# One product a tile for the group sums, one for turn and slots of kv, and both y halves of two experts at once

## The chip, the cores and the metric

The kernel runs on one core of one Trainium2 chip. The metric is device time in microseconds (us). A core has five engines that run side by side, each taking its own instructions in program order: PE (TensorE, matmuls into PSUM; PEld are its weight loads), DVE (VectorE), ACT (ScalarE), POOL (GpSimd) and SP (SyncE, which here issues nearly all transfers). They wait for each other on semaphores.

## The reference, cut to what matters

```python
kv  = einsum('bhsd,bhse->bhde', k, v)          # 8 batches, 8 heads, 576 rows, 64 wide
out = einsum('bhsd,bhde->bhse', q, kv)
x   = out / sqrt(mean(out*out, -1) + 1e-6) * g_norm     # -> 4608 tokens x 512
logits = x @ phi                                # 32 slots, 4 for each of 8 experts
d = softmax over tokens of logits;  slot_input = d.T @ x
h = relu(slot_input[e] @ w1[e]);  slot_out[e] = h @ w2[e]     # 512 -> 1024 -> 512
c = softmax over slots of logits;  return c @ slot_out
```

All operands are fp32. A matmul with fp32 operands shows in the trace as two instructions, which the text calls passes.

## The kernel before, in words

**Order.** The kernel writes out one program order by hand. `Order.add` records every operation with what it reads and writes, finds for each the operations on other engines that it must wait for, and `emit` gives them to the engines (so every instruction has line 214). In PSUM the unit of that bookkeeping is a whole bank: an operation that writes into a bank waits for every earlier read of that bank by another engine in the same 32 partitions. An engine never overtakes its own order.

**PSUM.** In the first phase the eight banks are shared out as `o` (two buffers of two banks, the products of a tile), `kv` (banks 4 and 5), `m` (one buffer, bank 6) and `s` (one buffer, bank 7). Tag `m` serves by turns `group_max_T` (the turned group maximum), `group_exp_PE` (the maximum spread to all partitions), the warm-up products of `fill_wide`, and `psT`.

**kv.** For each batch `Kv.products` and `Kv.borders` form k'v in PSUM, ACT copies it to `kvT`, and `Kv.slots` turns it (a transpose for each half g) and multiplies it with the gated phi (`gphi`, one matmul for each half). ACT copies both results into `bd`, the right operand of the next batches' products (for batch 0 DVE copies the second).

**Loop over 36 tiles of 128 tokens.** `products(T)` gives out and logits of a tile in one product with `bd`; ACT squares and copies it (`sq`, `part`, `xall`); DVE sums squares (`ms`), makes the inverse root with three small steps (`newton`) and adds the logits; POOL scales. Tiles form six groups G of six. When a group's logits are there, DVE takes their maximum (`group_max`), PE turns it (`group_max_T`), DVE reduces it (`group_max_row`), and two tiles later `group_exp` makes `d`. Then come `group_sum(G, i)` for i = 0, 2, 4, one in each of three tiles' turns. Each call multiplies d' with x of two tiles: four matmuls of 32 rows, two for the even and odd column blocks of each tile, one in each quarter of the output partitions, 258 columns each (two blocks of 128 and two ones columns, so that the sums of d come out too). After i = 4 DVE adds the result `pS` to `acc`, scaled by `alpha`.

**Tail.** After tile 35, groups 4 and 5 are left. The order there is: on DVE `group_max(G)` of the last group; then the sums of group 4 with their add into `acc`; then `fill_wide` (four matmuls of 512 fp32 columns, into tag `m`, whose result nobody reads); then `group_max_T`, `group_max_row`, `group_diag`, `group_exp` and the sums of group 5; then `psT`, which folds `acc` with `fold`, and the scaling into `sTe`.

**Experts and output.** `expert_h(e)` multiplies `sTe` with w1; `expert_y(e, hf)` multiplies the turned h with half hf of w2's columns (256) into bank hf of `pY`, eight matmuls of 32 rows in four quarters. After all `expert_y(e, 0)`, `gather(0)` copies the sums out, `mix(0)` adds the quarters with `sel`, and `output` forms the left half of the result and stores it; then the same for the right half. Weights stream in all through the kernel as their places become free.

Of the kernel before, what the change touches and what calls it, by code (L numbers as in the profile page):

```python
# [20 lines left out]
GROUPS = (6,) * 6  # L21
# [3 lines left out]
NX = 14  # L25
# [6 lines left out]
LATE = 6  # L32
# [253 lines left out]
def soft_moe_linear_attention(nc, first_in, kv_in, q0_in, q1_in, kv4_in, kv5_in, t3_in, w_in, out):  # L286


    const = Const(nc)
# [2 lines left out]
    arena = const.tile([P, HEAD + ARENA], F32, name="arena")  # L292
    phi_sb = arena[:, :128].rearrange("p (g w n) -> p g w n", g=2, w=2)
    g2 = arena[:, 128:129]
    xall = const.tile([P, NX, 4, 129], F32, name="xall")
    xflat = xall.rearrange("p i j n -> p (i j n)")


# [60 lines left out]

    nc.scalar.preload_act_table_set("natural_log_exp_and_others")  # L360

    ident = const.tile([P, P], F32, name="ident")
    make_identity(nc, ident)
    ones = const.tile([P, P], F32, name="ones")
    nc.gpsimd.memset(ones, 1.0)
    zeros = const.tile([P, 256], BF16, name="zeros")
    nc.vector.memset(zeros, 0.0)
    stepped = const.tile([P, 16], F32, name="stepped")
    small = const.tile([P, 4], F32, name="small")
    eps = small[:, :1]  # L370
    nc.gpsimd.memset(eps, EPS_RMS)
    fold = const.tile([P, 2, 64], F32, name="fold")
    nc.vector.tensor_reduce(out=fold[:, 0], in_=ident.rearrange("p (g n) -> p n g", g=2), axis=AX.X, op=ALU.add)
# [3 lines left out]
    gphi = const.tile([P, 2, 2, 2, NS], F32, name="gphi")  # L377
    nc.gpsimd.memset(gphi, 0.0)
    for i in range(2):
        lo = 64 * i  # L380
# [5 lines left out]
    nc.gpsimd.memset(xall[:, :, :, 128:129], 1.0)  # L386
    nc.gpsimd.tensor_copy(out=fold[:, 1], in_=fold[:, 0])
    xts = [xall[:, (i + 6) % NX] for i in range(NX)]

    L = const.tile([P, NT + len(GROUPS) + 1, NS], F32, name="logits")  # L390
# [2 lines left out]
        return T + T // GROUPS[0] + 1  # L393

    run_max = [small[:, 1 + i : 2 + i] for i in range(2)]
    acc = const.tile([P, 258], F32, name="acc")
# [4 lines left out]
    ps = pool(o=(2, 0, 2), kv=(2, 4), m=(1, 6), s=(1, 7))  # L401


    class Kv:


        def __init__(self, b, tag="kv", bufs=None):
            self.b = b
            self.bd = bds[b % 2]
            t = ps.tile([P, 2, 512], F32, tag=tag, name=f"kvp{b}_{tag}", bufs=bufs)  # L410
            self.pkv = t[:, :, :128].rearrange("p w (g d) -> p w g d", g=2)
            self.pT = t[:, 0, 128:384].rearrange("p (g n) -> p g n", g=2)
            self.pM = t[:, 1, 128:384].rearrange("p (g h w n) -> p g h w n", g=2, h=2, w=2)

        def products(self, r):
            g, w = divmod(r, 2)
# [30 lines left out]
        def slots(self, gs):  # L447
            kvT = [self.kvT[:, k].rearrange("p w d -> p (w d)") for k in range(len(gs))]
            for t, g in zip(kvT, gs):
                nc.tensor.transpose(self.pT[:, g], t, ident)  # L450
            for t, g in zip(kvT, gs):
                nc.tensor.matmul(self.pM[:, g], lhsT=t, rhs=gphi[:, g], start=True, stop=True)
            a, z = gs[0], gs[-1] + 1
            for i in range(2):
                lo = 64 * i
                nc.scalar.copy(
                    self.bd[lo : lo + 64, 2 * a : 2 * z, 32 + lo : 96 + lo],
                    self.pT[lo : lo + 64, a:z].rearrange("p g (h d) -> p (g h) d", h=2),
                )
# [123 lines left out]
    g0 = [sum(GROUPS[:G]) for G in range(len(GROUPS) + 1)]  # L583
# [37 lines left out]
    def group_exp(G):  # L621
# [6 lines left out]
        if G > 0:  # L628
            alphas[G] = wk.tile([P, 1], F32, tag="alpha", name=f"alpha{G}")
            nc.scalar.activation(alphas[G], run_max[G % 2], AF.Exp, scale=-1.0, bias=run_max[(G - 1) % 2])  # L630

    def group_sum(G, i):

        if i == 0:
            sums[G] = ps.tile([P, 258], F32, tag="s", name=f"pS{G}")
        pS = sums[G]
        for a in range(2):
            x = xts[(g0[G] + i + a) % NX]
            for j in range(2):
                at = 64 * a + 32 * j  # L640
                nc.tensor.matmul(
                    pS[at : at + 32].rearrange("p (j n) -> p j n", n=129),
                    lhsT=ds[G][:, i + a],
                    rhs=x[:, j::2],
                    start=i == 0,
                    stop=i == GROUPS[G] - 2,
                )
        if i == GROUPS[G] - 2:
            if G == 0:
                nc.vector.tensor_copy(out=acc, in_=pS)  # L650
            else:
# [32 lines left out]
    def fill(n, cols=256, home=None):  # L684

        if not n:
            return
        t = home if home is not None else ps.tile([P, 2, 512], F32, tag="o", name="fill", bufs=2)[:, 1]
        for i in range(n):
            nc.tensor.matmul(  # L690
                t[:, :cols].rearrange("p (a n) -> p a n", n=256),
                lhsT=zeros[:, :P],
                rhs=zeros.unsqueeze(1).to_broadcast([P, cols // 256, 256]),
                start=True,
                stop=True,
            )
# [26 lines left out]
    for T in range(NT - 2):  # L723
# [32 lines left out]
            group_exp_PE(pb_at[T])  # L756
            d_at[T + 1] = pb_at[T]
        if T in sums_at:
            todo_sums += [(sums_at[T], i) for i in range(0, GROUPS[sums_at[T]], 2)]
        if todo_sums:  # L760
            group_sum(*todo_sums.pop(0))
        if T in loads_behind:
# [12 lines left out]
    logits_adds(s - 2)  # L775
    scale_x(s - 2)
    group_exp(G - 1)
    todo_sums += [(G - 1, i) for i in range(0, GROUPS[G - 1], 2)]
    mean_square(s - 1)
    oZ = products(Z)  # L780
    root(s - 1, tail_ps[:, 0, 256 : 256 + H])
# [21 lines left out]
    group_exp(G)  # L803
    scale_o(Z, oZ, True)
    fill(LATE_FILL[2], home=tail_ps[:, 1], cols=512)
    for i in range(0, GROUPS[G], 2):
        group_sum(G, i)
    fill(LATE_FILL[3], home=tail_ps[:, 1], cols=512)

# [1 line left out]
    sTe = wk.tile([P, NE * 4 * NS], F32, tag="sq", name="sTe")  # L811
    nc.gpsimd.memset(sTe, 0.0)
    psT = ps.tile([P, P + 1], F32, tag="m", name="psT")
    for j in range(2):
        nc.tensor.matmul(
            psT[:, 64 * j : 64 * j + 64], lhsT=acc[:, 129 * j : 129 * j + 128], rhs=fold[:, 0], start=True, stop=True
        )
    nc.tensor.matmul(
        psT[:, 128:129], lhsT=fold.rearrange("p a n -> p (a n)"), rhs=acc[:, 128:129], start=True, stop=True
    )  # L820
    fill(LATE_FILL[4], home=tail_ps[:, 1], cols=512)
    mine = psT[:, :P].rearrange("p (j e k) -> p e j k", j=4, k=SPE)
# [37 lines left out]
    ]  # L860

    hTs = {}
    pY = ps.tile([P, 2, 512], F32, tag="y", name="pY", bufs=1)

    def w2_unit(e, hf):
        first = NE - LATE
        if e < first:
            return e, 8 * hf
        return first + hf * LATE // 2 + (e - first) // 2, 8 * (e % 2)

    def expert_h(e):
        ph = ps.tile([P, 2, 512], F32, tag="m", name=f"ph{e}")[:, 0, :256]
# [16 lines left out]
    def expert_y(e, hf, cs=range(8)):  # L889
        u, at = w2_unit(e, hf)  # L890
        for c in cs:
            j = c % 4
            nc.tensor.matmul(
                pY[32 * j : 32 * j + 32, hf, :256],
                lhsT=hTs[e][:, c],
                rhs=w_block("w2", u, at + c),
                start=e == 0 and c < 4,
                stop=e == NE - 1 and c >= 4,
            )

    zs = {}
# [3 lines left out]
    def halves(name, srcs):  # L907
        t = [wk.tile([P, 2, P], F32, tag="part", name=f"{name}_{f}", bufs=3)[:, f] for f in range(2)]
        nc.vector.tensor_copy(out=t[0], in_=srcs[0])
        nc.scalar.copy(t[1], srcs[1])  # L910
        return t

    def gather(hf):
        ys[hf] = halves(f"y{hf}", [pY[:, hf, f * P : f * P + P] for f in range(2)])

    def mix(hf):
        pz = [ps.tile([P, 2, 512], F32, tag="m", name=f"pz{hf}_{f}")[:, 0, :P] for f in range(2)]
        for f in range(2):
            nc.tensor.matmul(pz[f], lhsT=sel.rearrange("p a n -> p (a n)"), rhs=ys[hf][f], start=True, stop=True)
        zs[hf] = halves(f"z{hf}", pz)  # L920

    def step_over(n):
# [172 lines left out]
```

How the kernel before makes its waits and increments, by code:

```python
    def emit(self):  # L203
        nc = self.nc
        counters = {e: nc.alloc_semaphore(f"done_{e}") for e in ENGINES[:4]}
        sems = list(counters.values())
        counts = dict.fromkeys(counters, 0)
        for op in self.ops:
            method, args, kwargs = op.call
            engine = getattr(nc, op.engine)
            *before, last = sorted(op.waits, key=lambda w: w.i) or [None]
            for w in before:
                engine.wait_ge(w.sem, w.value)
            inst = getattr(engine, method)(*args, **kwargs)
            if last is not None:
                inst.wait_op(last.sem, last.value, "sem-ge")
            if op.dma:
                op.sem, op.value = nc.alloc_semaphore(f"dma_{op.i}"), 16
                sems.append(op.sem)
                inst.then_inc(op.sem, 16)
            elif op.signals:
                counts[op.engine] += 1
                op.sem, op.value = counters[op.engine], counts[op.engine]
                inst.then_inc(op.sem, 1)
        for op in self.ops:
            if op.dma and not op.signals:
                nc.sync.wait_ge(op.sem, 16)
        numbers = sorted(s.num for s in sems)
        assert numbers == list(range(numbers[0], numbers[-1] + 1))
        nc.sync.sem_clear(range(numbers[0], numbers[-1] + 1))
```

## Time and profile before

| | |
|---|---|
| time, median of 3 runs | 172.08 us (171.82 to 172.19) |
| time of the profiled execution | 171.97 us |
| its span, first to last instruction | 170.6 us |
| PE busy | 149.0 us (87%), 1832 instructions |
| DVE, ACT, POOL busy | 86.6, 89.0, 59.6 us |
| moved by DMA | 71.65 MB, 420 GB/s on the mean |

An engine's busy time is the union of its instructions' spans, and the spans of pipelined matmuls overlap, so the distance from one start to the next says what a matmul costs. Idle time of an engine is put down to what ended it.

### The profile page before, as it was taken

How to read it: one execution, taken by the hardware profiler on the slowest of the kernel's cores; microseconds unless marked ns; L12 is line 12 of the kernel's file. 1: busy time of each engine (PE TensorE's matmuls, PEld its weight loads, DVE VectorE, ACT ScalarE, POOL GpSimd, SP SyncE). 2: the span in 40 equal slices, each digit the busy share in tenths (PEclk: the TensorE clock that was granted, in tenths of full speed). 3: DMA queues.
4: the chain of work that ended last, by engine and by line, in shares of the span. 5: the costliest groups of instructions: out<-in, count | busy, mean ns of one | idle time of the engine just before them, and what ended most of it. 6: DMA issues, size and time to landing. Idle time of an engine off the chain costs nothing.

```text
span 170.6 us, 4233 instructions
## 1 busy us (share of the span) xinstructions
PE 149.0 (87%) x1832; PEld 105.0 (62%) x1832; DVE 86.6 (51%) x185; ACT 89.0 (52%) x230; POOL 59.6 (35%) x73
## 2 busy tenths in 40 slices
PE   7989696989999899999899998989999989989300
PEld 3468576979778888897697674346655543455000
DVE  1122156284677266762946698823888137218400
ACT  3027576796975886859759864202223045217400
POOL 7000707648357745377382679500000004000000
PEclk9999999999999999999999999999999999999955
DMA  5999999999999999999999999999999999999996
GB/s 186 417 429 421 444 415 439 473 416 452 462 415 421 432 441 430 419 399 451 415 449 407 455 392 421 447 434 415 430 426 442 436 442 392 431 419 434 416 455 277
DMA packets 4365, 71.65 MB, mean 420 GB/s; under 512 B 790, under 2 KB 790, under 8 KB 922
## 3 DMA queue, kind: packets, MB, share of 16 engines
q1 hardware_dynamic: 3994, 71.18, 97.8%
q8 instruction: 14, 0.23, 0.5%
q0 software_dynamic: 352, 0.20, 0.4%
q14 instruction: 5, 0.04, 0.1%
HBM read 61.94 MB, written 9.44 MB: 418 GB/s over the span
## 4 chain that ended last, share of the span: by engine, by line
PE 58%; DMA 13%; ACT 12%; DVE 7%; SPq 2%; issue 1%
PE psum L214 58%; DMA arena<-in_kv_dram 13%; ACT bd L214 3%; ACT sq L214 3%; ACT xall L214 2%; SPq L214 2%; DVE arena L214 1%; DVE logits L214 1%; ACT arena L214 1%; DVE ms L214 1%; ACT part L214 1%; ACT d L214 1%; DVE part L214 1%; ACT r L214 1%; DVE acc L214 1%
## 5 line engine op out<-in xcount | busy, mean ns | idle before, releaser
L214 PE MATMUL psum<-bd,arena 128*128 128x192 f32 (+1 forms) x320 | 56.1, 335 | 1.9 <-ACT bd L214 1.5
L214 PEld LDWEIGHTS psum<-bd,arena 128*128 128x128 f32 (+1 forms) x320 | 45.4, 179 | 8.7 <-ACT bd L214 2.8
L214 DVE TENSOR_REDUCE ms<-sq 128x16 f32<-128x1024 f32 (+1 forms) x19 | 22.1, 1162 | 32.8 <-ACT sq L214 32.5
L214 POOL TENSOR_TENSOR part<-part,r 128x512 f32<-128x512 f32 x17 | 17.8, 1048 | 49.6 <-DVE r L214 49.6
L214 POOL TENSOR_TENSOR xall<-xall,r 128x512 f32<-128x512 f32 x34 | 34.7, 1042 | 0.0
L214 ACT ACTIVATE sq<-psum 128x512 f32<-128x512 f32 x36 | 21.5, 598 | 11.7 <-PE psum L214 11.2
L214 PE MATMUL psum<-arena 128*64 128x64 f32 (+1 forms) x640 | 21.7, 226 | 2.8 <-DMA arena<-in_kv_dram 2.7
L214 PEld LDWEIGHTS psum<-arena 128*64 128x64 f32 (+1 forms) x640 | 19.0, 137 | 8.2 <-DMA arena<-in_kv_dram 3.6
L214 ACT COPY xall<-psum 128x512 f32<-128x512 f32 x34 | 20.6, 606 | 0.0
L214 ACT COPY part<-psum 128x256 f32<-128x256 f32 (+1 forms) x38 | 13.6, 359 | 11.2 <-DVE part L214 10.0
L214 DVE TENSOR_REDUCE logits<-part 128x64 f32<-128x512 f32 (+1 forms) x18 | 17.8, 988 | 0.0
L214 PE MATMUL psum<-logits,part 32*128 32x384 f32 x96 | 13.5, 523 | 1.5 <-ACT arena L214 0.7
L214 PE MATMUL psum<-arena,xall 128*32 128x256 f32 x256 | 14.7, 380 | 0.0
L214 ACT COPY arena<-psum 128x768 f32<-128x768 f32 (+1 forms) x14 | 10.2, 754 | 5.3 <-PE psum L214 5.2
L214 POOL DMA_DIRECT2D out_dram<-arena x2 | 1.2, 589 | 33.4 <-ACT arena L214 33.4
L214 PE MATMUL psum<-arena,sq 128*32 128x256 f32 x224 | 12.7, 379 | 0.2 <-DVE sq L214 0.2
L214 DVE COPY arena<-psum 128x768 f32<-128x768 f32 (+1 forms) x12 | 10.3, 888 | 4.7 <-PE psum L214 4.7
L214 PEld LDWEIGHTS psum<-arena,xall 128*32 128x32 f32 x256 | 8.3, 110 | 6.0 <-issue 1.0
L214 PE MATMUL psum<-xall,d 128*32 128x258 f32 x144 | 10.8, 390 | 0.8 <-ACT d L214 0.8
L214 PEld LDWEIGHTS psum<-logits,part 32*128 32x128 f32 x96 | 6.3, 183 | 7.8 <-ACT arena L214 4.3
L214 ACT COPY bd<-psum 64x128 f32<-64x128 f32 (+1 forms) x32 | 9.9, 309 | 1.6 <-PE psum L214 1.4
L214 PEld LDWEIGHTS psum<-arena,sq 128*32 128x32 f32 x224 | 7.2, 110 | 5.1 <-DVE sq L214 0.5
(80 smaller groups left out, 124.1 us busy)
## 6 DMA issues: line engine op xcount, KB each, us to landing
arena<-in_w_dram SPq DMA_DIRECT2D x4, 4096.0 KB, 23.5
arena<-in_w_dram SPq DMA_DIRECT2D x4, 2048.0 KB, 20.0
arena<-in_t_dram SPq DMA_DIRECT2D x1, 6912.0 KB, 36.1
arena<-in_w_dram SPq DMA_DIRECT2D x2, 3072.0 KB, 22.6
arena<-in_kv_dram SPq DMA_DIRECT2D x2, 2304.0 KB, 23.6
arena<-in_kv_dram SPq DMA_DIRECT2D x1, 4608.0 KB, 42.8
arena<-in_kv_dram SPq DMA_DIRECT2D x1, 3584.0 KB, 32.4
arena<-in_kv_dram SPq DMA_DIRECT2D x3, 1152.0 KB, 12.0
```

What stands on the lines that cost most here:

```text
L214: inst = getattr(engine, method)(*args, **kwargs)
```

## The change

- `xall` loses its ones columns (129 to 128 wide) and with them a memset; `fold` with its reduction and copy goes, and what used it uses `sel`.
- `group_sum` takes one matmul a tile: 32 rows, 512 columns, tile t of the group in quarter t % 4. It is called for i = 0 (four tiles) and i = 4 (two tiles). With i = 4 come three matmuls of two tiles' d (64 rows) with one column of ones into `p1`, a column of tag `m`. Then DVE adds `pS` (now 512 wide) to `acc` and `p1` to a column of `small`.
- `slots` makes turn and slots of a half in one matmul with `turns` (identity beside `gphi`), 256 columns, each half into a bank of its own.
- `psT` takes four matmuls of 32 columns with `sel` in place of two of 64 with `fold`; the one-column matmul stays.
- For experts 0 and 1 `expert_y` takes both halves in one matmul of 512 columns into bank 0; `gather_whole` copies that bank to SBUF on ACT; the other six experts go to bank 1 (hf 0) and bank 0 again (hf 1), and `mix` adds both parts with two matmuls where it had one.

```diff
-    xall = const.tile([P, NX, 4, 129], F32, name="xall")
+    xall = const.tile([P, NX, 4, P], F32, name="xall")
...
+    turns = const.tile([P, 3, P], F32, name="turns")
+    ident = turns[:, 0]
...
-                nc.tensor.transpose(self.pT[:, g], t, ident)
-            for t, g in zip(kvT, gs):
-                nc.tensor.matmul(self.pM[:, g], lhsT=t, rhs=gphi[:, g], start=True, stop=True)
+                nc.tensor.matmul(self.turned[:, g], lhsT=t, rhs=turns[:, : g + 2 : g + 1], start=True, stop=True)
...
+    def add_up(G, part, new):
+        if G == 0:
+            nc.vector.tensor_copy(out=part, in_=new)
+        else:
+            nc.vector.scalar_tensor_tensor(
+                out=part, in0=part, scalar=alphas[G], in1=new, op0=ALU.mult, op1=ALU.add
+            )
...
     def group_sum(G, i):
+        n = GROUPS[G]
         if i == 0:
-            sums[G] = ps.tile([P, 258], F32, tag="s", name=f"pS{G}")
+            sums[G] = ps.tile([P, 512], F32, tag="s", name=f"pS{G}")
         pS = sums[G]
-        for a in range(2):
-            x = xts[(g0[G] + i + a) % NX]
-            for j in range(2):
-                at = 64 * a + 32 * j
+        for t in range(i, min(i + 4, n)):
+            at = 32 * (t % 4)
+            nc.tensor.matmul(
+                pS[at : at + 32],
+                lhsT=ds[G][:, t],
+                rhs=xts[(g0[G] + t) % NX].rearrange("p j n -> p (j n)"),
+                start=i == 0,
+                stop=t + 4 >= n,
+            )
+        if i + 4 >= n:
+            p1 = ps.tile([P, P], F32, tag="m", name=f"p1{G}")[:, 64:65]
+            for t in range(0, n, 2):
+                at = t % 4 * 32
                 nc.tensor.matmul(
-                    pS[at : at + 32].rearrange("p (j n) -> p j n", n=129),
-                    lhsT=ds[G][:, i + a],
-                    rhs=x[:, j::2],
-                    start=i == 0,
-                    stop=i == GROUPS[G] - 2,
+                    p1[at : at + 64],
+                    lhsT=ds[G][:, t : t + 2].rearrange("p t n -> p (t n)"),
+                    rhs=ones[:, :1],
+                    start=t < 4,
+                    stop=t + 4 >= n,
                 )
...
+            add_up(G, acc, pS)
+            add_up(G, small[:, 4:], p1)
...
-    todo_sums += [(G - 1, i) for i in range(0, GROUPS[G - 1], 2)]
+    todo_sums += [(G - 1, i) for i in range(0, GROUPS[G - 1], 4)]
...
-    for j in range(2):
+    for j in range(4):
         nc.tensor.matmul(
-            psT[:, 64 * j : 64 * j + 64], lhsT=acc[:, 129 * j : 129 * j + 128], rhs=fold[:, 0], start=True, stop=True
+            psT[:, 32 * j : 32 * j + 32], lhsT=acc[:, P * j : P * j + P], rhs=sel[:, 0], start=True, stop=True
         )
...
+    def gather_whole():
+        nc.scalar.copy(y_whole, pY[:, 0])
...
-    expert_y(0, 0)
+    expert_y(0)
     combine(0)
     expert_h(2)
-    expert_y(1, 0)
+    expert_y(1)
+    gather_whole()
...
-    expert_y(0, 1)
-    expert_y(1, 1)
```

## Rows read from the trace of the kernel before

**Rows 1.** The page: busy time of each engine, and the main DMA queue.
```profile
PE 149.0 (87%) x1832; PEld 105.0 (62%) x1832; DVE 86.6 (51%) x185; ACT 89.0 (52%) x230; POOL 59.6 (35%) x73
...
q1 hardware_dynamic: 3994, 71.18, 97.8%
```

**Rows 2.** The page: the chain that ended last, by engine.
```profile
PE 58%; DMA 13%; ACT 12%; DVE 7%; SPq 2%; issue 1%
```

**Rows 3.** Timeline of PE from 22 to 36: start, us, instruction, [idle before <-what ended it].
```profile
26.88 1.15 PE L214 MATMUL psum<-arena 128*64 128x64 f32 x32 [1.34 <-DMA arena<-in_kv_dram]
```

**Rows 4.** Busy time by stretch: span, engines' busy us (instructions), clock, DMA share, GB/s.
```profile
60.00:102.00 42.00, 41.12 (x492) 33.26 (x491) 27.59 (x58) 32.53 (x91) 24.40 (x24) 1.00 0.99 426
```

**Rows 5.** The chain of waits from 98 to 115: start, us, what.
```profile
103.15 6.28 PE psum L214 x43
```

**Rows 6.** Timeline of PE from 93 to 118.
```profile
103.15 1.52 PE L214 MATMUL psum<-xall,d 128*32 128x258 f32 x24 [0.66 <-ACT d L214]
104.59 3.70 PE L214 MATMUL psum<-ones 128*128 128x512 f32 x8
108.24 0.42 PE L214 MATMUL psum<-ident,logits 128*32 128x128 f32 x8
...
112.81 0.66 PE L214 MATMUL psum<-fold,acc 128*128 128x64 f32 x4 [0.28 <-DVE acc L214]
113.30 0.33 PE L214 MATMUL psum<-acc,fold 128*128 128x1 f32 x2
113.50 0.38 PE L214 MATMUL psum<-zeros 128*128 128x512 bf16 x1
```

**Rows 7.** Timeline of DVE from 93 to 118.
```profile
107.64 0.55 DVE L214 TENSOR_REDUCE logits<-logits 128x32 f32<-128x224 f32 x1
108.11 0.47 DVE L214 SCALAR_TENSOR_TENSOR acc<-acc,alpha,psum 128x258 f32<-128x258 f32 x1
```

**Rows 8.** Groups by form: out<-in, shapes, count, busy us and mean ns.
```profile
L214 DVE TENSOR_TENSOR xall<-psum,r 128x512 f32<-128x512 f32 x2 | 1.4, 682 | 0.0
...
L214 DVE SCALAR_TENSOR_TENSOR r<-ms,psum 128x8 f32<-128x8 f32 x2 | 0.3, 164 | 0.6 <-ACT psum L214 0.5
```

**Rows 9.** Timeline of PE from 74 to 90.
```profile
76.37 0.38 PE L214 MATMUL psum<-ident,kvT 128*128 128x128 f32 x2
...
77.04 1.47 PE L214 MATMUL psum<-bd,arena 128*128 128x192 f32 x8
...
80.50 0.64 PE L214 MATMUL psum<-xall,d 128*32 128x258 f32 x8
81.08 1.57 PE L214 MATMUL psum<-bd,arena 128*128 128x192 f32 x8
83.23 0.49 PE L214 MATMUL psum<-ident,top 128*128 128x128 f32 x2 [0.59 <-DVE top L214]
```

**Rows 10.** Timeline of PE from 114 to 160.
```profile
129.63 7.27 PE L214 MATMUL psum<-arena,xall 128*32 128x256 f32 x128
137.30 0.79 PE L214 MATMUL psum<-part,sel 128*128 128x128 f32 x4 [0.40 <-DVE part L214]
```

**Rows 11.** Who waited for whom on PE: us in total, times, longest.
```profile
PE psum L214 <- ACT bd L214: 1.5, 3, 0.6
```

**Rows 12.** Busy time by stretch around PE's last matmul (columns as in rows 4).
```profile
159.00:160.00 1.00, 0.61 (x4) 0.00 (x0) 0.54 (x2) 0.66 (x2) 0.00 (x0) 1.00 1.13 479
...
162.00:163.00 1.00, 0.00 (x0) 0.00 (x0) 0.00 (x0) 0.00 (x0) 0.00 (x0) 0.60 1.21 516
```

**Rows 13.** Timeline of PE from 0 to 10.
```profile
1.06 2.31 PE L214 MATMUL psum<-zeros 128*128 128x512 bf16 x5 [1.06 <-DVE zeros L214]
3.16 2.89 PE L214 MATMUL psum<-ones 128*128 128x512 f32 x4
```

**Rows 14.** DMA issues: count, KB each, median us from issue to landing.
```profile
arena<-in_first_dram SPq DMA_DIRECT2D x1, 1224.0 KB, 5.4
out_dram<-arena SPq DMA_DIRECT2D x1, 3072.0 KB, 10.2
```

More of the change, by code:

```diff
@@ L360, in soft_moe_linear_attention @@
     nc.scalar.preload_act_table_set("natural_log_exp_and_others")
-    ident = const.tile([P, P], F32, name="ident")
+    turns = const.tile([P, 3, P], F32, name="turns")
+    ident = turns[:, 0]
     make_identity(nc, ident)
@@ L365, in soft_moe_linear_attention @@
     nc.gpsimd.memset(ones, 1.0)
-    zeros = const.tile([P, 256], BF16, name="zeros")
+    zeros = const.tile([P, P], BF16, name="zeros")
     nc.vector.memset(zeros, 0.0)
     stepped = const.tile([P, 16], F32, name="stepped")
-    small = const.tile([P, 4], F32, name="small")
+    small = const.tile([P, 5], F32, name="small")
     eps = small[:, :1]
     nc.gpsimd.memset(eps, EPS_RMS)
-    fold = const.tile([P, 2, 64], F32, name="fold")
-    nc.vector.tensor_reduce(out=fold[:, 0], in_=ident.rearrange("p (g n) -> p n g", g=2), axis=AX.X, op=ALU.add)
     sel = const.tile([P, 4, NS], F32, name="sel")
@@ L376, in soft_moe_linear_attention @@
     nc.gpsimd.tensor_copy(out=sel[:, 1:], in_=sel[:, :1].to_broadcast([P, 3, NS]))
-    gphi = const.tile([P, 2, 2, 2, NS], F32, name="gphi")
+    gphi = turns[:, 1:].rearrange("p g (h i n) -> p g h i n", h=2, i=2)
     nc.gpsimd.memset(gphi, 0.0)
@@ L385, in soft_moe_linear_attention @@
         nc.gpsimd.memset(bds[i], 0.0)
-    nc.gpsimd.memset(xall[:, :, :, 128:129], 1.0)
-    nc.gpsimd.tensor_copy(out=fold[:, 1], in_=fold[:, 0])
     xts = [xall[:, (i + 6) % NX] for i in range(NX)]
@@ L395, in soft_moe_linear_attention @@
     run_max = [small[:, 1 + i : 2 + i] for i in range(2)]
-    acc = const.tile([P, 258], F32, name="acc")
+    acc = const.tile([P, 512], F32, name="acc")
     def pool(**tags):
@@ L411, in __init__ @@
             self.pkv = t[:, :, :128].rearrange("p w (g d) -> p w g d", g=2)
-            self.pT = t[:, 0, 128:384].rearrange("p (g n) -> p g n", g=2)
-            self.pM = t[:, 1, 128:384].rearrange("p (g h w n) -> p g h w n", g=2, h=2, w=2)
+            self.turned = t[:, :, 128:384].rearrange("p g (a n) -> p g a n", a=2)
+            self.pT = t[:, :, 128:256]
+            self.pM = t[:, :, 256:384].rearrange("p g (h w n) -> p g h w n", h=2, w=2)
         def products(self, r):
@@ L456, in slots @@
                 nc.scalar.copy(
-                    self.bd[lo : lo + 64, 2 * a : 2 * z, 32 + lo : 96 + lo],
-                    self.pT[lo : lo + 64, a:z].rearrange("p g (h d) -> p (g h) d", h=2),
+                    self.bd[lo : lo + 64, 2 * a : 2 * z, 32 + lo : 96 + lo].rearrange("p (g h) d -> p g h d", h=2),
+                    self.pT[lo : lo + 64, a:z].rearrange("p g (h d) -> p g h d", h=2),
                 )
@@ L690, in fill @@
             nc.tensor.matmul(
-                t[:, :cols].rearrange("p (a n) -> p a n", n=256),
-                lhsT=zeros[:, :P],
-                rhs=zeros.unsqueeze(1).to_broadcast([P, cols // 256, 256]),
+                t[:, :cols].rearrange("p (a n) -> p a n", n=P),
+                lhsT=zeros,
+                rhs=zeros.unsqueeze(1).to_broadcast([P, cols // P, P]),
                 start=True,
@@ L758, in soft_moe_linear_attention @@
         if T in sums_at:
-            todo_sums += [(sums_at[T], i) for i in range(0, GROUPS[sums_at[T]], 2)]
+            todo_sums += [(sums_at[T], i) for i in range(0, GROUPS[sums_at[T]], 4)]
         if todo_sums:
@@ L805, in soft_moe_linear_attention @@
     fill(LATE_FILL[2], home=tail_ps[:, 1], cols=512)
-    for i in range(0, GROUPS[G], 2):
+    for i in range(0, GROUPS[G], 4):
         group_sum(G, i)
@@ L813, in soft_moe_linear_attention @@
     psT = ps.tile([P, P + 1], F32, tag="m", name="psT")
-    for j in range(2):
+    for j in range(4):
         nc.tensor.matmul(
-            psT[:, 64 * j : 64 * j + 64], lhsT=acc[:, 129 * j : 129 * j + 128], rhs=fold[:, 0], start=True, stop=True
+            psT[:, 32 * j : 32 * j + 32], lhsT=acc[:, P * j : P * j + P], rhs=sel[:, 0], start=True, stop=True
         )
     nc.tensor.matmul(
-        psT[:, 128:129], lhsT=fold.rearrange("p a n -> p (a n)"), rhs=acc[:, 128:129], start=True, stop=True
+        psT[:, 128:129], lhsT=sel.rearrange("p a n -> p (a n)"), rhs=small[:, 4:], start=True, stop=True
     )
@@ L862, in soft_moe_linear_attention @@
     hTs = {}
+    whole = NE - LATE
+    y_whole = xall[:, 8].rearrange("p j n -> p (j n)")
     pY = ps.tile([P, 2, 512], F32, tag="y", name="pY", bufs=1)
     def w2_unit(e, hf):
[L866 to L869, printed above, removed]
+        return whole + hf * LATE // 2 + (e - whole) // 2, 8 * (e % 2)
     def expert_h(e):
@@ L887, in expert_h, with expert_y @@
         nc.vector.transpose(out=hTs[e].rearrange("p c n -> p (c n)"), in_=h)
-    def expert_y(e, hf, cs=range(8)):
-        u, at = w2_unit(e, hf)
-        for c in cs:
+    def expert_y(e, hf=None):
+        for c in range(8):
             j = c % 4
[L893 to L899, printed above, removed]
+            if hf is None:
+                rhs = homes("w2", e)[0].rearrange("p (f n) -> p f n", f=2)[:, :, c * 256 : c * 256 + 256]
+                out = pY[32 * j : 32 * j + 32, 0].rearrange("p (f n) -> p f n", f=2)
+            else:
+                u, at = w2_unit(e, hf)
+                rhs = w_block("w2", u, at + c)
+                out = pY[32 * j : 32 * j + 32, 1 - hf, :256]
+            first, last = (0, whole - 1) if hf is None else (whole, NE - 1)
+            nc.tensor.matmul(out, lhsT=hTs[e][:, c], rhs=rhs, start=e == first and c < 4, stop=e == last and c >= 4)
     zs = {}
@@ L911, in halves @@
         return t
+    def gather_whole():
+        nc.scalar.copy(y_whole, pY[:, 0])
     def gather(hf):
-        ys[hf] = halves(f"y{hf}", [pY[:, hf, f * P : f * P + P] for f in range(2)])
+        ys[hf] = halves(f"y{hf}", [pY[:, 1 - hf, f * P : f * P + P] for f in range(2)])
     def mix(hf):
         pz = [ps.tile([P, 2, 512], F32, tag="m", name=f"pz{hf}_{f}")[:, 0, :P] for f in range(2)]
-        for f in range(2):
-            nc.tensor.matmul(pz[f], lhsT=sel.rearrange("p a n -> p (a n)"), rhs=ys[hf][f], start=True, stop=True)
+        for ready in (True, False):
+            for f in range(2):
+                y = y_whole[:, (2 * hf + f) * P : (2 * hf + f + 1) * P] if ready else ys[hf][f]
+                nc.tensor.matmul(pz[f], lhsT=sel.rearrange("p a n -> p (a n)"), rhs=y, start=ready, stop=not ready)
         zs[hf] = halves(f"z{hf}", pz)
```

7 lines of the change are left out of this document (removed).

## The prediction

> **What bounds the kernel now.** I read the page first, for who is busy: PE 149.0 of 170.6 us, the DMA queue 97.8% [rows 1]. Two resources look full, so the next view is the chain that ended last: 58% of it is PE and 13% DMA [rows 2]. The DMA part lies before 27 us, where PE waits 1.34 us for batch 2 [rows 3]; from there on the chain runs over PE, with short links of ACT and DVE. The stretch table says how tight: in the loop from 60 to 102 PE is busy 41.12 of 42.00 us [rows 4], so PE work that is added there is paid nearly in full. In the tail PE is filled on purpose: in the chain, PE from 103.15 runs 6.28 us over 43 instructions without a break [rows 5], and the timeline shows what they are: group 4's sums, then `fill_wide`, then the turned maximum [rows 6]. On DVE the last group's maximum starts at 107.64 and the add of group 4 at 108.11 [rows 7]. So `fill_wide` ends at 108.24 just as the maximum it bridges to is there. The transfers do not set the end: the last store takes 10.2 us from issue to landing [rows 14], and 3072 KB at the mean 420 GB/s are 7.5 us of that. So at most 2.7 us of it are queue and latency.
>
> **Group sums.** What a pass costs: 128 passes of 256 columns in quarters take 7.27 us, 0.057 each, four side by side, which is 0.23 for a quarter's 256 columns [rows 10]. Eight passes of 512 columns at full width take 3.65 us from start to start, 0.456 each [rows 6]. So the price goes by columns, also where quarters run side by side. A call of four matmuls (eight passes) before: 0.58 in the loop (80.50 to 81.08) [rows 9], 0.48 without other work between (24 passes in 1.44) [rows 6]; the difference, 0.10, is entering and leaving this shape. After: the call with four tiles is two passes of 512 columns in each quarter, 2 x 0.456 = 0.91, in the loop 1.01. The call with two tiles has the same two passes a quarter, but only in two quarters: again 1.01. If passes were priced singly (0.114) it would be 0.46 + 0.10; I take 1.01, since no row shows a quarter going through its columns faster. The three ones products are six passes of one column: two of them take 0.20 from 113.30 to 113.50 [rows 6], so 0.60 at most; at the 0.057 of quarter passes 0.34. I take 0.4, near the latter, since they too stand side by side. The Trainium skill (TensorEngine Tiling (Array Packing), section Performance Considerations) says that a matmul carries some 60 cycles of overhead, so that one column costs as much as sixty. By that page six passes would be an estimated 0.15 us and the sum 1.0 us lower; the row with 0.10 a pass speaks against it. In the loop a group goes from 3 x 0.58 = 1.74 to 2.42, +0.68. Groups 0 to 3: **+2.7** (0.7 with the low prices).
>
> **Slots.** Before, 76.37 to 77.04, 0.67 [rows 9]. After, four passes of 256 columns at full width, 4 x 0.228 = 0.91: +0.24, six times behind 27 us, 1.4. Behind three of the slots steps PE waits for `bd` anyway, 1.5 us in all [rows 11], and absorbs the extra: **+0.7** (0 to 1.4). ACT can no longer begin with the turned half while PE does the slots, since both halves' banks hold both, but ACT still has the tile's square and two copies to do before.
>
> **DVE's add in the loop** grows from 0.47 to some 0.7 (a 512-wide operation from PSUM: 682 ns) plus the small one, 0.16 [rows 7, 8]. It also moves one tile earlier, ahead of the next group's `group_max_T`, which writes into tag `m`, where `p1` is being read. At 83.23 PE already waits 0.59 there for DVE [rows 9]; the add then lengthens that wait, but the third call no longer follows it: I count nothing net (0 to +0.9 over four groups).
>
> **The tail, the largest term.** `p1` of group 4 stands in tag `m`, the one bank into which `fill_wide` writes next. So `fill_wide` must wait until DVE has read `p1`. That add is in DVE's order behind `group_max` of the last group and behind the 512-wide add. In the times of before: the adds begin at 108.11, take 0.68 + 0.16, and end at 108.95 [rows 7, 8]; PE begins `fill_wide` at 109.0 instead of 104.59. Behind it in PE's order stand its 3.65 us and then `group_max_T`, and for that wait in turn `group_max_row`, `group_diag`, `group_exp` and all the rest. A filler that bridged the wait now follows it: **+4.4** (3.9 if half a microsecond of DVE's chain comes sooner; 4.8 with a wider add). Group 4's own longer sums, to 105.45, vanish in this wait; PE stands idle for some 3.55 us.
>
> **Rest of the tail.** Group 5: `pS` is ready after 1.82 instead of 1.44 [rows 6], +0.4; the add +0.2; the small add that `psT` now also waits for, in the same bank, +0.16; `psT` with four more passes at 0.12 (112.81 to 113.30 are four) [rows 6], +0.5. Together **+1.3** (0.6 to 1.6).
>
> **Experts.** `expert_y` of two experts costs the same columns; nothing (-0.2 if 32 instructions fewer matter). `gather_whole` is one more ACT copy, in a stretch in which ACT mostly waits for PE. `mix` gets four more passes a half, which PE can do in the 0.40 in which it waits for the gather [rows 10]: **+0.1** (0 to 0.6). The lost memset, `fold` and the narrower zeros lie before 27 us, covered by the wait for batch 2 [rows 3]: nothing, and if uncovered a gain below those 1.34 us.
>
> **Last store.** PE comes later, so the queue ahead of it is shorter. The first load, 1224 KB, landed 5.4 us after issue on an empty queue; 3.0 are its bytes, 2.4 the rest [rows 14]. So the store alone needs 7.5 + 2.4 = 9.9 of its 10.2: **-0.3** (-2.7 to 0).
>
> **The sum at full clock**: 2.7 + 0.7 + 4.4 + 1.3 + 0.1 - 0.3 = +8.9, on the execution's own 171.97 us (1.37 beyond its span of 170.6, and 0.1 under the median 172.08): 180.9.
>
> **The clock.** PE's last matmul ends at 159.61, and in the slice from 162 the granted clock is 0.60 on the mean, so it fell at about 162.2, 2.6 us after PE went idle, from 2.4 to 1.2 GHz [rows 12]. The new idle time in the tail is 3.55 us, longer. If the clock falls there, `fill_wide` runs at the lower level until it returns. All eight passes at half speed would lose another 3.65; at the span's start five short and four wide passes were through by 6.05, five us after the first, the four wide ones in 2.89 where eight later take 3.65 [rows 13, 6], so the return takes less than five us of work. I take half of 3.65, **+1.9**: 182.8. The Trainium skill (TensorE: Matmul & The Clock Gate, section Why this matters for your kernels) states that a gap of this order between bursts of matmuls brings PE back to half clock. By that rule the time is the 182.8; without it, the 180.9. The row of the fall at the span's end agrees with the rule.
>
> **Rivals.**
> 1. *The clock holds through the stall* (chance 0.28): 180.9. For it: no row shows a fall in so short a gap between two bursts. Against: 2.6 us were enough once.
> 2. *Passes are priced singly, not by columns* (0.12): the second call costs 0.46 + 0.10 and the ones products 0.34 or less, so groups 0 to 3 cost +0.7 and slots, with two passes fewer, nothing. The tail's wait stays: 0.7 + 4.4 + 0.8 - 0.3 = +5.6 and 0 to 1.9 of clock: 177.6 to 179.5. Against it: 0.057 in quarters and 0.456 at full width for twice the columns [rows 10, 6].
> 3. *The transfers set the end, so PE's delay is covered* (0.04): the queue is 97.8% busy [rows 1]. Then 172, not slower. It decides only while PE's delay stays under what the last store spends queued, at most 2.7 us by the numbers above, 0.3 by the nearer row; the tail's wait alone is beyond it.
> 4. *The stall starves more than the tail* (0.08): PE's delay also holds back the weight loads that wait for it, the queue runs dry, and the experts wait: 185 to 188.
>
> My forecast, with the clock falling, has 0.48. The range reaches from rival 2's lower part to the forecast with nearly the whole fill at half speed and loop terms at their upper ends: 177.5 to 186.5. About 0.2% (0.35 us) is what a measurement of this kernel tells from no change; faster by more than that 0.01, within it 0.03 (both rival 3), slower 0.96.
>
> **What would show it.** Right: in the profile after, an idle stretch of PE of 3 to 4 us just ahead of `fill_wide`, released by DVE's add into `small`; the granted clock below 1.00 in the slices behind it; sums calls of about 1.0 us in the loop; `group_max_T` of the last group 7 to 10 us later than 108.24. Wrong: `fill_wide` following the sums directly, calls of four 512-column matmuls near 0.6, or PE waits for weights between 120 and 150.

## The result, and the profile after

The changed kernel takes 183.11 us (median of 4 runs, 182.76 to 183.35) against 172.13 before: 1.0643 times as long, 95% interval 1.063 to 1.0655. The profiled execution took 183.35 us with a span of 182.0, 11.4 more than before. The page after: busy time by engine, the main DMA queue, and the chain that ended last.

```profile
PE 159.1 (87%) x1760; PEld 108.2 (59%) x1760; DVE 88.1 (48%) x190; ACT 89.9 (49%) x231; POOL 59.3 (33%) x71
...
q1 hardware_dynamic: 3994, 71.18, 92.6%
...
PE 57%; DMA 13%; DVE 12%; ACT 10%; SPq 2%; issue 1%
```

Against [rows 1, 2] PE has 72 instructions fewer and 10 us more to do, DVE's share of the chain has gone from 7% to 12%, and the DMA queue is no longer full. Where the chain now passes over DVE shows in the timeline of PE in the tail (start, us, instruction, idle before it and what ended it):

```profile
105.83 1.91 PE L214 MATMUL psum<-xall,d 128*32 128x512 f32 x12 [0.81 <-ACT d L214]
107.67 0.39 PE L214 MATMUL psum<-ones,d 128*64 128x1 f32 x6
111.68 5.40 PE L214 MATMUL psum<-ones 128*128 128x512 f32 x8 [3.62 <-DVE small L214]
117.01 0.43 PE L214 MATMUL psum<-turns,logits 128*32 128x128 f32 x8
...
119.45 1.91 PE L214 MATMUL psum<-xall,d 128*32 128x512 f32 x12 [0.19 <-ACT d L214]
...
122.34 1.08 PE L214 MATMUL psum<-sel,acc 128*128 128x32 f32 x8 [0.33 <-DVE small L214]
```

and in that of DVE beside it:

```profile
110.31 0.54 DVE L214 TENSOR_REDUCE logits<-logits 128x32 f32<-128x224 f32 x1
110.77 0.74 DVE L214 SCALAR_TENSOR_TENSOR acc<-acc,alpha,psum 128x512 f32<-128x512 f32 x1
111.42 0.21 DVE L214 SCALAR_TENSOR_TENSOR small<-small,alpha,psum 128x1 f32<-128x1 f32 x1
```

Group 4's sums begin 2.68 later than in [rows 6] (103.15), and `fill_wide` 7.09 later (104.59): PE stands idle for 3.62 us until DVE has done the maximum of the last group, the wide add and the small one. Then it takes 5.33 from start to the next start, where it took 3.65. The maximum that `fill_wide` was to bridge to is there at 110.85 (110.31 + 0.54), and PE turns it at 117.01: of these 6.16 us the filler alone takes 5.33. The stretches of that place (columns as in rows 4) tell why it is so slow:

```profile
110.00:111.00 1.00, 0.00 (x0) 0.00 (x0) 0.97 (x3) 0.00 (x0) 1.00 (x2) 1.00 0.92 385
111.00:112.00 1.00, 0.32 (x1) 0.30 (x2) 0.63 (x2) 0.00 (x0) 0.53 (x1) 1.00 1.08 451
112.00:113.00 1.00, 1.00 (x2) 0.34 (x1) 0.00 (x0) 0.00 (x0) 0.00 (x0) 0.53 1.18 508
...
115.00:116.00 1.00, 1.00 (x3) 0.45 (x2) 0.00 (x0) 0.00 (x0) 0.00 (x0) 0.76 0.98 418
...
121.00:126.00 5.00, 4.48 (x56) 2.81 (x58) 1.58 (x6) 0.00 (x0) 0.00 (x0) 1.00 0.28 121
```

The granted clock goes from its upper level (1.00) to the lower (0.50) just after `fill_wide` has begun, and comes back between 115 and 116. The last line shows the DMA queue running dry, 0.28 busy: SP, which waits for PE before it issues, sends the next weight load only at 126.04. PE never waited for a weight load.

In the loop, the timeline of PE at the place of [rows 9]:

```profile
77.69 1.03 PE L214 MATMUL psum<-turns,kvT 128*128 128x256 f32 x4
78.55 1.46 PE L214 MATMUL psum<-bd,arena 128*128 128x192 f32 x8
...
82.44 1.05 PE L214 MATMUL psum<-xall,d 128*32 128x512 f32 x4
83.42 0.39 PE L214 MATMUL psum<-ones,d 128*64 128x1 f32 x6
83.74 1.57 PE L214 MATMUL psum<-bd,arena 128*128 128x192 f32 x8
85.84 0.49 PE L214 MATMUL psum<-turns,top 128*128 128x128 f32 x2 [0.53 <-DVE small L214]
```

This slots step takes 0.86 (0.67 before); the six behind 27 us take 0.86 to 0.97 (0.66 to 0.72 before), 1.36 more in all. PE's wait for `bd`, 1.5 us in three places before [rows 11], has shrunk by 0.7:

```profile
PE psum L214 <- ACT bd L214: 0.8, 2, 0.5
```

Its wait for DVE in the loop has grown: 0.53 here and 0.39 at 101.70, where the kernel before has only the 0.59 of [rows 9]. A call with only two tiles takes 0.98, as long as one with four (1.00, 79.94 to 80.94), and the six one-column passes 0.32. And one stretch that nothing had announced, in the second half's `expert_y`, first PE's timeline and then the stretches:

```profile
156.37 7.07 PE L214 MATMUL psum<-arena,xall 128*32 128x256 f32 x96
163.38 0.71 PE L214 MATMUL psum<-xall,sel 128*128 128x128 f32 x4
```

```profile
156.00:157.00 1.00, 1.00 (x10) 0.40 (x12) 0.00 (x0) 0.48 (x1) 0.00 (x0) 0.72 1.05 381
157.00:158.00 1.00, 1.00 (x14) 0.42 (x8) 0.00 (x0) 0.00 (x0) 0.00 (x0) 0.50 1.00 418
```

The same 96 passes took 5.39 us before; the clock has fallen a second time. The last store is issued at 171.75, 11.48 later than before (160.27), and takes 10.1 to land, about as before (10.2):

```profile
out_dram<-arena SPq DMA_DIRECT2D x1, 3072.0 KB, 10.1
```

So the profiled execution's 11.38 us come to: loop 2.7 (to group 4's start), wait 4.4 (111.68 - 105.83 = 5.85 in place of 1.44; group 4's longer sums lie inside it), clock in `fill_wide` 1.7 (5.33 - 3.65), rest of the tail 1.2 (from 119.45 to the experts' start at 124.04, 4.59; before 110.68 to 114.06, 3.38), experts -0.2, second fall of the clock 1.7, store -0.1.

### The profile page after: what moved, and what is told of

The parts are those of the page before. It is cut to its first block, busy times and chain, and to the rows that moved or that the text cites. A ratio compares the mean times of both kernels' runs of the same rounds, so it can differ in the third digit from the quotient of the medians.

```text
span 182.0 us, 4092 instructions
## 1 busy us (share of the span) xinstructions
PE 159.1 (87%) x1760; PEld 108.2 (59%) x1760; DVE 88.1 (48%) x190; ACT 89.9 (49%) x231; POOL 59.3 (33%) x71
## 4 chain that ended last, share of the span: by engine, by line
PE 57%; DMA 13%; DVE 12%; ACT 10%; SPq 2%; issue 1%
PE psum L214 57%; DMA arena<-in_kv_dram 13%; DVE logits L214 3%; DVE ms L214 3%; ACT bd L214 3%; ACT sq L214 2%; SPq L214 2%; DVE arena L214 1%; ACT xall L214 1%; ACT arena L214 1%; DVE r L214 1%; DVE acc L214 1%; DVE part L214 1%; ACT part L214 1%; DVE small L214 1%
## 5 line engine op out<-in xcount | busy, mean ns | idle before, releaser
L214 PEld LDWEIGHTS psum<-bd,arena 128*128 128x128 f32 (+1 forms) x320 | 46.3, 179 | 7.1 <-ACT xall L214 2.0
L214 ACT COPY xall<-psum 128x512 f32<-128x512 f32 x35 | 21.2, 605 | 1.2 <-PE psum L214 1.2
L214 PE MATMUL psum<-arena,xall 128*32 128x256 f32 (+1 forms) x224 | 16.2, 446 | 0.0
L214 PE MATMUL psum<-xall,d 128*32 128x512 f32 x72 | 12.3, 603 | 1.0 <-ACT d L214 1.0
L214 ACT COPY arena<-psum 128x768 f32<-128x768 f32 (+1 forms) x14 | 10.2, 754 | 5.3 <-PE psum L214 5.2
L214 PE MATMUL psum<-ones 128*128 128x512 f32 x12 | 8.8, 899 | 3.6 <-DVE small L214 3.6
L214 PEld LDWEIGHTS psum<-arena,xall 128*32 128x32 f32 x224 | 7.8, 120 | 7.1 <-issue 3.5
```

Source lines behind the costliest of these rows:

```text
L214: inst = getattr(engine, method)(*args, **kwargs)
```

## The experiments

**The wait taken out.** Group 4's ones column goes into the one tail bank that is free there.

```diff
-            p1 = ps.tile([P, P], F32, tag="m", name=f"p1{G}")[:, 64:65]
+            if G == len(GROUPS) - 2:
+                p1 = tail_ps[:, 1, :1]
+            else:
+                p1 = ps.tile([P, P], F32, tag="m", name=f"p1{G}")[:, 64:65]
```

> The change as it is, but the ones column of group 4 goes into a bank that nothing else uses at that point, so that fill_wide need not wait for DVE. Theory (the shared bank holds PE back 4.4 us and its idle time drops the clock, 1.7 us): 183.1 - 4.4 - 1.7 = 177.0 with the granted clock 1.00 from 108 to 118; 175.3 if the second fall of the clock, at 156, goes too. Rival (DVE's longer adds and PE's longer sums make the tail late whatever the bank): 180 or more.

176.81 us (4 runs: 175.82, 175.98, 177.65, 177.76). Its PE timeline:

```profile
105.62 1.91 PE L214 MATMUL psum<-xall,d 128*32 128x512 f32 x12 [0.80 <-ACT d L214]
107.46 0.39 PE L214 MATMUL psum<-ones,d 128*64 128x1 f32 x6
107.78 3.70 PE L214 MATMUL psum<-ones 128*128 128x512 f32 x8
111.41 0.42 PE L214 MATMUL psum<-turns,logits 128*32 128x128 f32 x8
```

`fill_wide` follows the sums at once and takes 3.63 at full clock; the turned maximum comes at 111.41 in place of 117.01. The two pairs of times are 1.8 us apart, and go with the mean granted clock: 0.973 and 0.978 in the short ones, 0.966 in the long ones, one of them the profiled one, where the second fall is at 151. Expected were 177.0 and 175.3; both pairs lie 0.5 to 0.8 above. The traces give the reason: without the wait, group 4's sums (105.62 to 107.78, 2.16 in place of 1.44) are no longer hidden in it. So of the 5.85 us between the sums' start and `fill_wide` the shared bank costs 3.7, and the longer sums take 0.7. The rival falls, and the second fall of the clock comes in some executions only.

**The wait kept, PE busy in it.**

```diff
+    fill(16, home=tail_ps[:, 1], cols=512)
     fill_wide(ps.tile([P, 512], F32, tag="m", name="fill"), LATE_FILL[0])
```

> The change as it is, with 16 short bf16 products on zeros between the sums of group 4 and fill_wide, into a bank of their own, so that PE is busy through most of its wait for DVE. Theory (the wait costs 4.4, the clock's fall in it another 1.7): fill_wide still begins near 111.7 but takes 3.65 instead of 5.33, time 181.4. Rival (the clock falls or fill_wide runs slowly for another reason than the idle time): 183.1, fill_wide still 5.3 us. If the fall at 156 hangs on when the first one was, it may move as well: 179.7.

179.22 us (178.09 to 180.39). PE's timeline:

```profile
107.51 3.63 PE L214 MATMUL psum<-zeros 128*128 128x512 bf16 x16
111.23 3.70 PE L214 MATMUL psum<-ones 128*128 128x512 f32 x8
114.86 0.43 PE L214 MATMUL psum<-turns,logits 128*32 128x128 f32 x8
```

The granted clock of the whole span in 40 slices of 4.5 us (tenths, 9 is 0.9 or more):

```profile
PEclk9999999999999999999999999999999999799965
```

`fill_wide` begins as late behind the sums as in the changed kernel (5.88 behind their start at 105.35) and takes 3.63 at full clock in place of 5.33. So the wait and the clock are two prices, and with PE kept busy the clock does not fall there: the first slice below 9 is the 35th, from 152. Expected were 181.4, or 179.7 if the second fall moved. Three of the four executions (178.09 to 179.22) have a mean clock of 0.978 to 0.981, which fits no second fall; the profiled one, 180.39, has it at 154. This one is 2.96 below the changed kernel's: 1.70 is the clock in `fill_wide`, 0.48 an earlier start of group 4 (105.35 for 105.83, with the same loop), and 0.9 the last store, which took 9.2.

**The wait alone, in the kernel before.** One word: `fill_wide` writes into the bank that DVE's add of group 4 reads.

```diff
-    fill_wide(ps.tile([P, 512], F32, tag="m", name="fill"), LATE_FILL[0])
+    fill_wide(ps.tile([P, 512], F32, tag="s", name="fill"), LATE_FILL[0])
```

> The kernel before with one word changed: fill_wide writes into tag s, the bank of group 4's sums, in place of tag m, so that it must wait for DVE's add of group 4 as it does in the changed kernel; no other part of the change. Theory (a filler behind the wait that it should bridge): fill_wide begins near 108.6 in place of 104.6, +4.0, the clock falls in the idle time, +1.7, the store's slack takes 1.4 back: 176.4, or 174.7 if the clock holds. Rival (the wait costs so much only with the longer sums and adds): under 174.

176.28 us, 1.0255 of the kernel before (1.0222 to 1.0288). PE's timeline:

```profile
103.40 1.52 PE L214 MATMUL psum<-xall,d 128*32 128x258 f32 x24 [0.66 <-ACT d L214]
108.88 5.40 PE L214 MATMUL psum<-ones 128*128 128x512 f32 x8 [3.96 <-DVE acc L214]
114.20 0.43 PE L214 MATMUL psum<-ident,logits 128*32 128x128 f32 x8
```

A stretch in the middle of `fill_wide`, its clock at 0.50:

```profile
111.00:112.00 1.00, 1.00 (x2) 0.34 (x1) 0.00 (x0) 0.00 (x0) 0.00 (x0) 0.50 1.10 475
```

3.96 us of idle time, 5.32 of `fill_wide` and the lower clock in it, without any part of the change: the rival falls.

**Slots as before in the changed kernel, and slots alone in the kernel before.**

The edit of the first, less the lines that place the results in the banks; the second makes the opposite edit in the kernel before.

```diff
...
-                nc.tensor.matmul(self.turned[:, g], lhsT=t, rhs=turns[:, : g + 2 : g + 1], start=True, stop=True)
+                nc.tensor.transpose(self.pT[:, g], t, ident)
+            for t, g in zip(kvT, gs):
+                nc.tensor.matmul(self.pM[:, g], lhsT=t, rhs=turns[:, 1 + g], start=True, stop=True)
```

> The change with turn and slots of kv as before (transposes, then the products with gphi, each kind into one bank). Theory (passes are priced by columns, half of the extra is absorbed by waits for bd): slots steps of 0.67 instead of 0.87 to 0.94, time 0.5 to 0.7 lower, 182.5. Rival (ACT's later begin on both banks delays the products of the next batch): 1.4 lower or more, 181.7. Rival (ACT sets that stretch and nothing of it is paid): 183.1.

> The kernel before with turn and slots of kv in one product, nothing else. Theory (0.2 us more for each of six steps, half absorbed by waits for bd): 172.05 + 0.6 = 172.6, at most 173.3. Rival (ACT sets that stretch): 172.05. Rival (fewer instructions pay): 171.8.

The first takes 181.60 us (181.25 to 182.10), 1.5 less than the changed kernel; the second 172.00 us, ratio 0.9999 (0.999 to 1.0007). The first is at the value of its first rival (181.7), but its profile does not bear that rival out: with the old slots PE waits 1.5 us for `bd`, with the new ones 0.8, so the new ones do not lengthen that wait. It has group 4's sums at 105.35, 0.48 earlier than the changed kernel; but the run with the busy wait, which has the new slots, has them at 105.35 too. The last store took 8.7 us in place of 10.1, and that is most of the difference between the two profiled executions (181.31 and 183.35). In the second, group 4's sums start at 103.41, 0.26 later than before; but in the run with the wait alone, whose loop is that of the kernel before, they start at 103.40. So executions of one loop differ by nearly as much as the slots were to cost, and neither run shows a cost of them that reaches the tail.

**Experts alone in the kernel before** (`expert_y(0)`, `expert_y(1)`, `gather_whole` and `mix` of the change).

> The kernel before with only the experts' part of the change: both halves of experts 0 and 1 in one product, the copy of their bank, two more products in each mix. Theory (same columns, the extra products of mix run while PE waits for the gather; the clock's fall at 156 comes from where the stages fall in time, not from this part): 0.1 to 0.2 under the kernel before, 171.9, clock 1.00 until PE's end. Rival (the new order of the output stage lets the clock fall there): 173.8, a fall between 139 and 152.

171.96 us, ratio 1.0 (0.9991 to 1.0009); neither gain nor loss shows, and the profiled execution has the clock at 1.00 until PE's end. The runs that follow tell why little could show here: PE has some 1.4 us to spare in the kernel before.

**The kernel before, 1.8 us later.**

```diff
-LATE_FILL = (4, 3, 3, 1, 1)
+LATE_FILL = (6, 3, 3, 1, 1)
```

> The kernel before with six products in fill_wide in place of four, nothing else: all that follows lies 1.8 us later. Theory (the clock's fall in the output stage hangs on when that stage comes, and not on what the change did there): 172.05 + 1.8 = 173.9, and in some executions another 1.7, 175.6, with a fall near the end of the first half's output, as at 156 in the changed kernel. Rival (the fall comes from the changed kernel's own work): 173.9 in every execution.

172.46 us (172.11 to 173.71, 12 runs), ratio 1.0031 (1.0015 to 1.0047). Both theories had 173.9, and both were wrong there: PE's turned maximum stood at 109.85 in place of 108.24, and the last store was issued at 161.72 in place of 160.27, but landed after 8.9 us in place of 10.2:

```profile
out_dram<-arena SPq DMA_DIRECT2D x1, 3072.0 KB, 8.9
```

Two of the 12 executions, 173.34 and 173.71, have a mean clock of 0.968 and 0.969; the others have 0.974 or more.

**Three calls of the sums in one turn, in the kernel before.**

```diff
-        if todo_sums:
+        while todo_sums:
             group_sum(*todo_sums.pop(0))
```

> The kernel before with all three calls of group_sum in one tile's turn, nothing else. Theory (entering and leaving the shape of 32-row products costs 0.10 us each time): three calls back to back take 1.54 in place of 3 x 0.58 = 1.74, 0.2 for each of four groups: 171.25. Rival (PE's longer absence in that turn leaves ACT without a tile and is paid there): 172.05 or more.

172.04 us, ratio 1.0 (0.9991 to 1.0008). The three calls took 1.44 back to back (46.33 to 47.77), 0.10 less than expected. With one call at 0.58, that is an estimated 0.43 a call and 0.15 for entering and leaving the shape. The experts begin at 113.54 in place of 114.06, but PE then waits 0.42 us for a weight load (at 134.88), where the kernel before waits for none. The profiled execution shows by chance why nothing can be seen of such gains. The stretches, and its last store (KB, us to landing):

```profile
146.00:147.00 1.00, 1.00 (x6) 0.20 (x8) 0.07 (x1) 0.23 (x1) 0.00 (x0) 0.64 1.05 442
147.00:148.00 1.00, 1.00 (x16) 0.45 (x12) 0.00 (x0) 0.25 (x1) 0.00 (x0) 0.50 0.98 402
```

```profile
out_dram<-arena SPq DMA_DIRECT2D x1, 3072.0 KB, 8.7
```

Here too the clock fell at 146, PE's last output began at 160.26 in place of 158.69, and the time was 172.01: the store made it up.

**Fewer bytes.** The kernel before without its last weight load.

```diff
...
-    ("w2", 2): (32, 120), ("w2", 3): (72,), ("w2", 4): (88,), ("w2", 5): (0,), ("w2", 6): (16,), ("w2", 7): (56,),
+    ("w2", 2): (32, 120), ("w2", 3): (72,), ("w2", 4): (88,), ("w2", 5): (0,), ("w2", 6): (16,), ("w2", 7): (16,),
...
-        if e == 5:
-            load_w("w2", 7)
```

> The kernel before without its last weight load (2048 KB of w2, the right half of experts 6 and 7); those products read the unit before it instead, so the output's right half leaves out that part. PE's work is the same. Theory (in the kernel before the transfers set the end, and PE's last output comes 1.4 us before it would have to): the last store finds an empty queue and lands 8.7 to 9 us after issue, 170.7. Rival (PE sets the end, as the prediction had it): 171.8 to 172.05, the store still some 10 us.

170.56 us, ratio 0.9914 (0.9899 to 0.993), with PE's work as it was and its last store issued at 160.06, 0.21 earlier than before. The store:

```profile
out_dram<-arena SPq DMA_DIRECT2D x1, 3072.0 KB, 8.7
```

So in the kernel before the transfers set the end, and PE has some 1.4 us to spare. The kernel before's own executions agree: their mean clock goes from 0.968 to 0.978, as in kernels with and without the second fall, and their times stay within 171.8 and 172.4.

**The last store in two.** `(8, 9, 10, 11)` becomes `(8, 9), (10, 11)`.

> The kernel before with its last store of four chunks in two of two chunks each, the first issued as soon as its chunks are there. Theory (the queue is full to the end, so an earlier issue of half of it gains only the short gap ahead of it): 171.8 to 172.05. Rival (the last store's own size and latency set the end, behind PE): PE ends at 160.3 and 1536 KB and latency take some 5 us less than 3072 KB: 168 to 170.

172.16 us, ratio 1.0007 (0.9998 to 1.0016): an earlier issue gains nothing, as expected with a full queue. In its profile, too, the clock fell at 146, with PE's program unchanged.

**Sums alone, without the wait, and with all four quarters in use.** The second kernel multiplies the two last tiles of a group in halves (against the changed kernel):

```diff
...
-        for t in range(i, min(i + 4, n)):
-            at = 32 * (t % 4)
+        for k in range(4):
+            t, cols = (k, slice(0, 512)) if i == 0 else (4 + k // 2, slice(k % 2 * 256, k % 2 * 256 + 256))
             nc.tensor.matmul(
-                pS[at : at + 32],
+                pS[32 * k : 32 * k + 32, cols],
...
```

> The kernel before with the group sums' part alone (one product a tile, ones products, psT with sel), and the ones column of group 4 in a bank of its own, so without the wait. Theory (passes are priced by columns): loop calls 1.00 + 0.99 + 0.32 in place of 3 x 0.58, 0.57 a group, group 4 0.5 and the tail 1.2 more: 172.05 + 2.3 + 0.5 + 1.2 = 176.0, less what waits in the loop absorb (to 175.0). Rival (passes are priced singly, 18 for 24): 172.5 or less.

> As the kernel with the sums' part alone and no wait (f3), but the two last tiles of a group are multiplied in halves of 256 columns over all four quarters. Theory (a call costs its quarters' columns, so two idle quarters are what made the sums dear): the second call falls from 0.99 to 0.57, 0.42 for each of six groups, 2.5 less PE time; 175.1 - 2.5 = 172.6, less where the store's own slack covers it (172.2). Rival (the calls are paid by passes, four more here): 175.1 or more.

The first takes 175.13 us: 174.26 and 174.31 at a mean clock of 0.978 and 0.982, 175.95 (the profiled one, with a fall at 150) and 176.06 at 0.970 and 0.966. The second takes 174.54 (174.32 to 174.94). PE's timeline, a line of the first and then the second:

```profile
118.06 3.66 PE L214 MATMUL psum<-arena,sq 128*32 128x256 f32 x64 [0.19 <-DVE sq L214]
```

```profile
97.22 0.64 PE L214 MATMUL psum<-xall,d 128*32 128x256 f32 x8
97.79 0.39 PE L214 MATMUL psum<-ones,d 128*64 128x1 f32 x6
...
116.63 5.35 PE L214 MATMUL psum<-arena,sq 128*32 128x256 f32 x64 [0.19 <-DVE sq L214]
```

The call with two tiles takes 0.57 in place of 0.99 with four passes more: columns in a quarter set the price, as expected. The experts begin at 116.63 in place of 118.06, 1.43 earlier, not 2.5; part of what PE saved in the loop turned into waits for DVE (0.80 at 100.48 in place of 0.40 at 101.12). In the second kernel the clock fell at 117, in the first 64 passes of the experts (5.35 in place of 3.66), and not again in the output stage; all four executions have a mean clock of 0.966 to 0.968. So its fair match is the first kernel's pair with a fall, 175.95 and 176.06, and against these it gains 1.0 to 1.7, about the 1.43 of PE; against the pair without one it gains nothing. No version that computes the same and beats the kernel before came out.

## Why the prediction was right, and where it was not

The forecast was 182.8 with the clock falling, the result 183.11, and the four signs named for it all came: 3.62 us of idle time ahead of `fill_wide`, released by DVE's add into `small`; the lower clock behind it; calls of 0.98 to 1.00; `group_max_T` 8.77 later. The main terms, wait and clock, were right in mechanism and size. That the sum came so close is partly luck: a second fall of the clock, 1.7 us, was in no term, and loop, clock, tail and experts together were charged some 1.3 us too much.

- **Group sums**: right in kind, 0.57 a group (1.00 + 0.99 + 0.32 - 1.74) for the forecast 0.68. The one-column passes cost 0.053 each, where 0.067 was taken. The Trainium skill (TensorEngine Tiling (Array Packing), section Performance Considerations) would have them at the estimated 0.15 for six; the trace has 0.32. Passes priced singly (rival 2) is out: the calls of two and of four tiles cost the same. One reading was inconsistent: the 24 passes in 1.44, taken as free of entering and leaving the shape, contain one entry and one exit. The three calls in one turn put these at an estimated 0.15, not 0.10; it changes little here.
- **Slots**: 0.23 a step for 0.24, and the waits for `bd` absorbed 0.7 of the 1.36, as forecast. Whether the remaining 0.7 reached the tail is not shown: group 4 came 0.26 later with slots alone, and executions of an unchanged loop differ by up to 0.6 there (102.77 to 103.40).
- **DVE's add in the loop**: PE's waits for DVE grew by some 0.3, where nothing net was counted. Loop, slots and this add together: 2.7 for 3.4.
- **The wait**: 4.41 for 4.4, by the mechanism forecast. Taking the bank away gives 3.7 of it back, since the other 0.7 is group 4's longer sums, which the prediction let vanish in the wait; these end, by the prediction's own terms, at 105.37 (103.15 + 1.82 + 0.4) and not 105.45. In the kernel before, the wait alone costs 4.04 on PE.
- **The clock in it**: 1.68 for 1.9. Rival 1 is out for this kernel. The Trainium skill (TensorE: Matmul & The Clock Gate, section Why this matters for your kernels) says that such a gap brings half clock; the trace agrees, with the fall just behind 3.62 us of idle time. The prediction's bound on the clock's return rests on the durations of passes in [rows 13] alone: the granted clock reads 1.00 there, from 0 to 7. In `fill_wide` itself the stretches show both the fall and the return.
- **Rest of the tail**: 1.2 for 1.3. **Experts**: -0.2 for +0.1, and alone not measurable.
- **What failed, first**: "The transfers do not set the end" and with it the last store's -0.3. The step took the price of a store on an empty queue from a load (9.9 us) and so found only 0.3 of slack. Measured on an emptier queue it is 8.7 to 8.9 (the kernel before 1.8 us later, with three calls, with fewer bytes), and fewer bytes with the same PE work gave 170.56. In the sum this cost only 0.2, because the store of the changed kernel again took 10.1. Rival 3 was right about the kernel before; what it can cover, put there between 0.3 and 2.7, is some 1.4 us, far below PE's delay. That fits slots, experts and three calls alone, which cost or gain nothing. In the changed kernel's own profile the queue had run nearly empty ahead of the last two stores; in the kernel with the old slots, where it had too, the last one took 8.7. Why it varies is open.
- **What failed, second**: the second fall of the clock, 1.7 us, was in no term. It is not the change's own work: it shows in the kernel before with three calls in one turn and in the one with the split store (at 146 in both), in the one with the sums alone, and by the mean clock the same program has it in some executions and not in others. In the kernel before PE's spare 1.4 us can swallow most of it; in the changed kernel nothing is left to swallow it. That it hangs on where the stages fall in time was the theory; what decides it was not isolated.
- **Rival 4**: the queue did run dry (0.28 busy from 121 to 126), but PE waited for no weights.
- **Not tried**: the changed kernel without `fill_wide`. With the filler behind the wait, 5.33 us of its work stand between the maximum and its turn; what would be left without it is not shown.

## What to carry to other kernels

A temporary that borrows a buffer inherits the buffer's next writer: before putting a new result into a shared bank, look for who writes there next, and what stands ahead of its reader on the reader's engine. Work that only fills a wait has to stand ahead of that wait; behind it, it is paid in full. Products side by side in quarters were paid here by the columns of the fullest quarter (0.98 us for two tiles, 1.00 for four, 0.57 for two spread over four quarters), so fewer and wider products that leave quarters idle cost time. Where two resources end close together, as PE and the transfers did here, a change on one shows nothing until it has used up the slack: the wait alone put PE's last output 5.80 us later (164.49 for 158.69) and the profiled execution's time 4.44 (176.41 for 171.97).

## What the runs showed of the hardware that was not expected

The clock fell in stretches where PE never stood idle for more than fractions of a microsecond (at 146, 151, 154, 156 in the output stage, at 117 as the experts began; the longest of these idle times is 0.42), about 1.7 us lost where it can be compared, and, by the mean clock, in some executions of a kernel but not in others. The last store, 3072 KB, took between 8.7 and 10.2 us, and 8.7 and 10.1 in two kernels whose queue had run nearly empty ahead of the last two stores.
